# One transfer instead of six for the mixing weights, and final chunk outputs issued inside a pair of products

## The reference

```python
# stage 1: recurrence over 768 steps, 4 batches x 8 heads, 40 x 40 state
y[:, :, t] = einsum('bhd,bhde->bhe', rt, state)
Sa = einsum('bhde,bhe->bhd', state, at)
state = state * wt[:, :, None, :] - einsum('bhd,bhe->bhde', Sa, bt) + einsum('bhd,bhe->bhde', vt, kt)
# stage 2: x = y as (4, 768, 320)
h = relu(x @ w_in); u, v = h[..., :512], h[..., 512:]
v_n = (v - mean(v)) / sqrt(var(v) + 1e-6)
x = (u * (einsum('ts,bsd->btd', w_spatial, v_n) + b_spatial[None, :, None])) @ w_out
# stage 3: one of 8 experts for each token (argmax gate, kept from the token before by a local gate)
out[b, s] = p[e] * (relu(x[b, s] @ w1[e]) @ w2[e])
```

## Time and profile before

| | |
|---|---|
| three launches | 937.5, 935.6, 935.27 us; median 935.6 |
| the profiled one of them | 937.5 us, of which the span from first to last instruction is 935.7 |
| TensorE busy | 918.3 us, 98% of the span |
| DVE, POOL, ACT busy | 477.4, 255.9, 250.9 us |
| granted TensorE clock, mean | 0.99 |

### The profile page before, as it was taken

The page is one execution under the profiler, slowest core; times in us unless marked ns, Lnnn a source line. Parts: engine busy times, 40 slices in busy tenths (PEclk is TensorE's granted clock), DMA queues, the critical chain, the costliest instruction groups (busy, mean ns, idle before and its releaser), DMA issues.

```text
span 935.7 us, 54057 instructions
## 1 busy us (share of the span) xinstructions
PE 918.3 (98%) x24653; PEld 712.3 (76%) x24654; DVE 477.4 (51%) x1026; ACT 250.9 (27%) x527; POOL 255.9 (27%) x231
## 2 busy tenths in 40 slices
PE   6999999999999999999999999999999999999997
PEld 6899999999999975555555555568888888888885
DVE  5477777787778643645355455463352222222220
ACT  0244444444444422102102112112212121212220
POOL 6454555545554551000020020020350111111011
PEclk8999999999999998999999999999999999999999
DMA  4235554554344321960110110339221110001100
GB/s 118 81 113 174 155 174 151 156 158 141 108 148 131 106 60 33 314 193 1 51 43 1 51 43 0 95 93 333 66 99 37 31 42 29 25 28 35 29 30 4
DMA packets 61477, 86.01 MB, mean 92 GB/s; under 512 B 22786, under 2 KB 41038, under 8 KB 61424
## 3 DMA queue, kind: packets, MB, share of 16 engines
q1 hardware_dynamic: 37232, 63.30, 22.6%
q10 hardware_dynamic: 21168, 13.32, 5.3%
q0 software_dynamic: 3024, 8.72, 2.6%
HBM read 72.47 MB, written 14.45 MB: 93 GB/s over the span
## 4 chain that ended last, share of the span: by engine, by line
PE 98%; issue 1%; DMA 0%; ACT 0%; DVE 0%; POOL 0%; SPq 0%; DVEq 0%; POOLq 0%; ACTq 0%
PE ps_D L1588 14%; PE ps_D L288 8%; PE ps_G L1570 6%; PE ps_E L1570 6%; PE ps_B L300 6%; PE ps_E L1078 5%; PE ps_A L288 4%; PE ps_B L206 3%; PE ps_G L1577 3%; PE ps_D L1113 3%; PE ps_D L1050 3%; PE ps_E L1076 3%; PE ps_G L206 3%; PE ps_E L206 3%; PE ps_D L1152 2%; PE ps_A L1055 2%
## 5 line engine op out<-in xcount | busy, mean ns | idle before, releaser
L1588 PE MATMUL ps_D<-room,hT 128*128 x496 | 138.9, 433 | 0.0
L1588 PEld LDWEIGHTS ps_D<-room,hT 128*128 128x128 f32 x496 | 91.9, 190 | 34.8
L1531 POOL DMA_INDIRECT out<-y,token x31 | 34.8, 1123 | 255.2 <-DVE y L1696 183.9
L644 POOL DMA_INDIRECT sorted_rows<-rows,slot x24 | 23.9, 994 | 237.7 <-DVE slot L636 231.6
L1696 DVE TENSOR_SCALAR y<-ps_D,x_in 128x320 f32<-128x320 f32 x31 | 17.1, 550 | 125.5 <-PE ps_D L1588 125.5
L1632 ACT ACTIVATE hT<-ps_G 128x512 f32<-128x512 f32 x31 | 18.5, 598 | 216.5 <-PE ps_E L1577 216.5
L1679 DVE COPY w_own<-room 128x1024 f32 x62 | 44.3, 720 | 62.9 <-PE ps_G L1570 34.3
L1328 DVE STREAM_TRANSPOSE room<-room 128x256 f32<-128x256 f32 x96 | 42.3, 441 | 47.7 <-ACT room L1217 47.7
L1570 PEld LDWEIGHTS ps_G<-xTt,w_own 128*128 128x128 f32 x496 | 59.9, 192 | 5.6 <-issue 1.3
L1570 PE MATMUL ps_G<-xTt,w_own 128*128 128x128 f32 x496 | 60.7, 276 | 0.6 <-ACT hT L1632 0.6
L1570 PE MATMUL ps_E<-xTt,w_own 128*128 128x128 f32 x496 | 60.4, 275 | 0.0
(11 more groups left out here) (256 smaller groups left out, 1773.6 us busy)
## 6 DMA issues: line engine op xcount, KB each, us to landing
room<-in_moe_w SPq DMA_DIRECT2D x8, 1280.0 KB, 14.1
room<-in_moe_w SPq DMA_DIRECT2D x8, 1024.0 KB, 11.4
room<-in_vt SPq DMA_DIRECT2D x24, 320.0 KB, 3.8
room<-in_kb SPq DMA_DIRECT2D x46, 160.0 KB
x_in<-sorted_rows ACTq DMA_DIRECT2D x27, 161.0 KB, 2.2
room<-in_vo SPq DMA_DIRECT2D x24, 160.0 KB, 4.0
room<-in_rg SPq DMA_DIRECT2D x48, 80.0 KB
room<-in_r SPq DMA_DIRECT2D x48, 80.0 KB
```

Source lines behind the costliest of these rows:

```text
L1531: pool.indirect_dma_start(out=self.out[:, :], out_offset=bass.IndirectOffsetOnAxis(ap=side.token[:, u:u + 1], axis=0), in_=side.y[:, u % 2 ...
L1588: mm = pe.matmul(self.ps_y[:, u % 2], side.hT[:, u % 2, f, :], self.weights.w2[:, bass.ds(e, 1), f, :], start=(f == 0), stop=(f == self.NF ...
```

## The change

The six tiles of w_spatial become one transfer, so ACT's schedule of loads has 5 calls of the first kind (chunks 1 to 5) and `load_out` runs in chunks 6 to 15. In the passage, `scores_r` moves ahead of `values(0, 2)`, and the last `outputs`, with its two waits, moves between the two tiles' products of `values(0, 2)`. In `values`, batch 0 waits for both tiles of x ahead of the first product; before, it waited for the second tile behind the first tile's products.

```diff
-        self.transfers = TILES + 1 + NK
+        self.transfers = 2 + NK
...
-        pairs = [(self.wspT[:, t, :], w_spatial[t * P:(t + 1) * P, :]) for t in range(TILES)]
+        pairs = [(self.wspT[:, :, :], w_spatial.rearrange("(t p) s -> p t s", p=P))]
...
     def values(self, pe, b, i, between=None):
 
-        if b == 0:
-            pe.wait_ge(self.x_tile[i], 16 * (NK + 1))
+        for t in (i, i + 1):
+            if b == 0:
+                pe.wait_ge(self.x_tile[t], 16 * (NK + 1))
         if b >= 1 and i == 0:
             pe.wait_ge(self.x_full, 16 * (NK + 1) * b)
-
-        def second():
-            if between:
-                between()
-            if b == 0:
-                pe.wait_ge(self.x_tile[i + 1], 16 * (NK + 1))
-
         self.pair(pe, self.v_at(b, i), D_HALF,
                   lambda g, k, rows: self.xT[rows, k, (i + g) * P:(i + g + 1) * P],
-                  lambda g, k, rows: self.win[rows, k, D_HALF:], second)
+                  lambda g, k, rows: self.win[rows, k, D_HALF:], between)
...
                 gated.fold(pe, woutT, wgl, A[:, 1].rearrange("p (d n) -> p d n", n=P), folded)
-                gated.values(pe, 0, 2, lambda: scores_r(now))
-                pe.wait_ge(kt_d, CHUNKS)
-                pe.wait_ge(rvu_d, now)
-                outputs(now)
+                scores_r(now)
+
+                def final_outputs():
+                    pe.wait_ge(kt_d, CHUNKS)
+                    pe.wait_ge(rvu_d, now)
+                    outputs(now)
+
+                gated.values(pe, 0, 2, final_outputs)
                 gated.gates(pe, 0, 0)
```

## The result

The changed kernel takes 941.43 us (median of five launches, 939.7 to 943.19) against 935.62 us for the kernel before beside it: ratio 1.0062, 95% interval 1.0047 to 1.0078, 5.8 us slower. I had forecast no change, 935.9 us.

What follows compares the result with a forecast made beforehand. The prediction took TensorE, 98% of the span, as the bound. Its terms 0 + 0.3 + 0.0 + 0 gave +0.3 us on the 935.6 us median, so 935.9 us, range 933.8 to 938.0.

Steps and rivals of the forecast that it cites:

- The view of the bound: Whole kernel: TensorE is 98% of the chain of waits; other edits count only by changing a wait of TensorE.
- Part 1, the calls that go: Stage 1, ACT's queue: five issues of some 0.36 us removed where TensorE does not wait for ACT; 0 us.
- the crowd in chunk 1: Stage 1, pass c = 1: five further tiles fill DMA engines to 11.3 of 12 us, delaying rg; +0.3 us, range 0 to 3.8.
- rival D: Stage 1, c = 1: rg lands behind the one large load, stall of 3.8 us, 939.4 us; 6%.
- Part 2, the order of the passage: Passage from the fold to gates: same instructions reordered, no new waits, gates(0, 0) starts at 365.08 against 365.06; 0.0 us.
- The low stretch: Passage: TensorE's clock at half for about 6.9 us, from 1 to 2 us behind the fold, in both orders.
- A: Passage: the clock comes back sooner, after 3.4 us at half; 1.7 us gained, 934.2 us; 12%.
- B: Passage: the clock does not fall; -3.3 us, 932.6 us; 6%.
- C: Passage: the clock is low for 3.4 us longer; +1.7 us, 937.6 us; 6%.
- slower: Whole kernel: the outcome of a measurably slower time, beyond about 0.3% or 2.8 us; 9%.
- Part 3, the wait for both tiles: values(0, 4): tile 5 of x lands 2.9 us ahead of need as outputs ends 4.0 us earlier; 0 us.
- Rival E: values(0, 4): the upfront wait bites since the store's chain does not move forward; +1.1 us, some 937.0 us; 6%.

Runs made afterwards that it cites:

- e2: Changed kernel with the six separate w_spatial loads of before, so only the new passage order and early wait for x's tiles; 937.32 us, ratio 0.9999.
- e7: e1 with rg's load issued some 8 us earlier in each of SP's chunks; 936.42 us, ratio 0.9993 of the kernel before.
- e12: e1 with the joined load issued in chunk 21 instead of chunk 1; 937.72 us, ratio 1.0004 of the kernel before.
- e6: e1 with the joined load issued by SP, on rg's own queue, in chunk 1; 943.33 us, ratio 1.0072 of the kernel before.
- e1: Kernel before with the joined w_spatial load alone, passage order as before; 943.24 us, ratio 1.0058.
- e11: e1 with the joined load as two transfers of 384 columns each, both in chunk 1; 943.49 us, ratio 1.0063 of the kernel before.
- e13: Kernel before with 22 short extra ACT copies ahead of its turned-state copy in chunk 2, no large load; 945.16 us, ratio 1.0078.
- e3: Kernel before with w_spatial in two loads of 1152 KB, in chunks 1 and 2, order as before; 939.79 us, ratio 1.002.
- e9: Kernel before with 11 extra ACT copies of 128 columns ahead of its turned-state copy in chunk 2, no large load; 941.76 us, ratio 1.0041.
- e4: e1 with the joined load issued some 10 us later, at the end of ACT's chunk 1, behind rg's issue; 940.26 us, ratio 1.0033 of the kernel before.

## Why the prediction was wrong

**The view of the bound** was right: TensorE at 98%, and nothing off it counts but by a wait. The waits the change removes were already met; e2's ratio of 0.9999 says so.

**Part 1, the calls that go.** Worth 0, as forecast: e7 and e12 have five calls fewer and are not measurably faster, and the one issue that stays took 0.45 us, near the lower end of my 0.36 to 2.2. The joined load even did land in 13.4 us where six loads took 4.8 us each, 28.8 in sum. By the Trainium skill (DMA: Bandwidth & Descriptors, Rules for kernel authors) small transfers should be joined, and at the page's fixed cost an estimated 10 us of transfer time would come back. Nothing of it reached the end of this kernel, since nothing waited for w_spatial.

**Part 1, the crowd in chunk 1. This is the step that failed.** The sum was right as a sum: 6.2 + 5.1 = 11.3 us of engine time, and 0.84 x 12 = 10.1 us were spent by 68 us and the rest by 71. The value taken from its range was not: I took 0.3 us of 0 to 3.8, "near the lower end, because ... rg is on SP's and w_spatial on ACT's" queue. Measured are 2.75 us, and e6 shows the reason given to be void, since rg's own queue is as good or bad. What the traces show in its place is that both queues' packets share the engines, so that all of SP's loads were slowed; when rg was issued, 0.49 MB of its own queue stood ahead of it, where it had been 0.09. I had set those loads aside with "needed a pass later" and "several us of room": they had room, but rg was behind them.

Two more things belong to the step. 11.3 of 12 us is a mean over 16 engines, and the loads of 40 rows (w, r, rg) kept only 66% of them at work, so those engines had more to do than the mean. And slack of 0.58 us is small beside any such difference; with the engines full up to the time of rg's issue, the higher end of the range was the nearer row. The Trainium skill's rule of turns between queues (same page, Queues, rings and completion order) was the better guide. I read it as "slowed to about half speed and not put behind the backlog"; the trace agrees with the turns (71.2% and 29.3% of the engines' time at once, from 60 to 67 us), and a transfer slowed by them still waits for what its own queue has ahead of it.

**What an idle TensorE costs.** A second fault of the same step, and of rival D, which had the place and the wait, if not whose backlog it was: I priced a stall by its own length. D at 3.8 us gave 939.4; it came as a stall of 2.75 us and 941.4. In e1 5.8 us (3.5 to 7.3) were lost with 2.8 of stall. The excess of low-clock time, 22.3 - 13.2 = 9.1 us, is worth at most 4.5 us, if all of it fell on work that runs at half speed. It is likely to be less: among the 77 launches of the kernel before, 10 us more of low-clock time went with about 2 us more of run time, which would make it an estimated 2 of the other 3 us. That an idle time can let the clock fall is shown by e11 and e13; how much of the 5.8 us is clock is not. I had the price of the low clock in my hands, in the passage, and looked for it there alone.

**Part 2, the order of the passage.** Forecast 0.0; measured 20.87 us against 20.93, and ratio 0.9999 alone. The low stretch lasted 6.8 us in the trace after, as laid out, but it began within the fold and not 1 to 2 us behind it, so that the layout came out right in its sum and not row by row. Its length looks like chance: it was 6.8 us before and after, 3.4 in e2, e3 and e12, 10.2 in e9, and missing in e4, with the same fold. So rivals A, B and C were no alternatives between two kernels but more likely the scatter of each: the kernel before went from 935.0 to 940.9 us, and a trace at one length was too little to weigh them by.

**Part 3, the wait for both tiles.** 0, right. `outputs` ended 365.57 - 347.68 = 17.9 us behind the passage's first group, before it was 20.9: 3.0 us earlier and not 4.0, since the clock fell elsewhere. Tile 5's last load was issued at 371.65, and with the 2.1 us of the earlier trace rows it landed 2.0 us ahead of its use (forecast 2.9). Rival E did not come.

**Chances.** Only 6% for D and 9% for slower was too little for a load that fills 11.3 of 12 us in front of a slack of 0.58.

## What to carry to other kernels

Before loads are joined, look at what small transfer is issued while the joined load is under way (some 13 us here) with someone waiting for it, at its slack, and at what its own queue has ahead of it, since all of that is slowed too. The joined load is free where the transfer is early enough (e7) or its queue has little else to carry (e12), and a queue of its own is no protection (e6). A mean share of the DMA engines near 1 up to the deadline is to be read as a likely miss, not as a fit, above all when the transfer in question does not use all 16 engines. And an idle time of TensorE in a kernel that keeps it 98% busy can cost more than its length: by the medians, e4 lost 2.9 us for 2.25 us of further idle time in its trace (1.3 times), e1 5.8 for 2.8 (twice), e13 8.1 for 3.1 (2.6 times).

## What the runs showed of the hardware that I had not expected

- Idle times of TensorE of 2.4, 3.2 and 3.1 us were followed by about 3.4 us at half clock in the profiles of e6, e11 and e13, and not in those of e1 and of the kernel after, with 2.7 us. Over many launches the low-clock time rose from about 13 to 18 to 22 us in these five kernels.
- An issue on ACT's queue took 4.70 us instead of some 0.4 in e6, 3.2 us after the large load on SP's queue had landed, and two stores 2.96 us instead of some 1 us right behind the issue of 1152 KB on ACT's own (e3). What holds an issue up is not shown. The issuing engine stands still meanwhile, and so does what is behind on its list.
- A transfer issued 0.01 us ahead of a 2304 KB one (e4) was ready for its copy 4.9 us after its issue, 2.6 us in the kernel before. From 67 to 70 us the two queues took 74.8% and 19.3% of the engines' time.
- Loads of 40 rows kept 66% of the 16 engines at work when nothing else was under way (e6, 68 to 69.5 us), a load of 128 rows all of them.
